# A 128-byte array in front of a fused attention and expert kernel's hid values

## The reference

```python
p = domain_probs / (domain_probs.sum(-1, keepdims=True) + 1e-09)
for e in range(E):
    h = np.maximum(x @ w1[e], 0.0)
    out += p[:, e:e + 1] * (h @ w2[e])
...
h = x @ w_in
g = h * np.cos(h)
return g @ w_out
```

## The kernel before

| array | first byte before | past a multiple of 256 | first byte after | past a multiple of 256 |
|---|---|---|---|---|
| w_hi, w_lo | 16512, 49280 | 128 | same | 128 |
| w_raw, x_hi, x_lo | 82048, 98432, 116864 | 128 | same | 128 |
| hp_hi | 135488 | 64 | 135616 | 192 |
| hp_lo | 141632 | 64 | 141760 | 192 |
| h_raw | 147776 | 64 | 147904 | 192 |
| ident, acc | 153984, 156544 | 128 | 154112, 156672 | 0 |
| t_hi, t_lo | 174976, 184192 | 128 | 175104, 184320 | 0 |
| ex_hi, ex_lo | 193408, 209792 | 128 | 193536, 209920 | 0 |
| attention's q_t, k_t, v_w, prob, prob_t; the cosine's c_u to c_cos | 174976 and on | 128 | 128 more | 0 |

## Time and profile before

### The profile page before, as it was taken

The page is one execution under the profiler, slowest core; times in us unless marked ns, Lnnn a source line. Parts: engine busy times, 40 slices in busy tenths (PEclk is TensorE's granted clock), DMA queues, the critical chain, the costliest instruction groups (busy, mean ns, idle before and its releaser), DMA issues.

```text
span 638.2 us, 10145 instructions
## 1 busy us (share of the span) xinstructions
PE 628.9 (99%) x3656; PEld 562.1 (88%) x3656; DVE 304.4 (48%) x722; ACT 259.6 (41%) x554; POOL 272.9 (43%) x404
## 2 busy tenths in 40 slices
PE   6999999999999999999999999999999999999997
PEld 5887899999899999999998888889999999999996
DVE  6754431215433315433315433426775666766564
ACT  6775322233321223321223321246555467544542
POOL 6883236698720296720296720287000059400000
PEclk9999999999999999999999999999999999999999
DMA  9864100012220021210022210033100002001011
GB/s 281 277 211 153 58 0 1 1 51 82 66 67 1 1 66 66 66 66 0 1 66 67 67 66 1 21 112 100 34 0 1 1 36 98 1 0 49 0 51 50
DMA packets 21896, 37.25 MB, mean 58 GB/s; under 512 B 2784, under 2 KB 14048, under 8 KB 21856
## 3 DMA queue, kind: packets, MB, share of 16 engines
q1 hardware_dynamic: 20688, 36.71, 17.7%
q10 hardware_dynamic: 1168, 0.02, 0.1%
HBM read 34.36 MB, written 2.36 MB: 58 GB/s over the span
## 4 chain that ended last, share of the span: by engine, by line
PE 96%; DVE 2%; ACT 1%; issue 1%; POOL 0%; DVEq 0%
PE bank L1194 31%; PE bank L1166 31%; PE bank L1225 16%; PE bank L1211 14%; PE bank L1158 2%; PE bank L1142 1%; PE bank L1122 1%; DVE s_sb L823 1%; PE bank L1308 1%; ACT prob L574 1%; PE bank L1350 1%; DVE acc L973 0%; DVE prob_t L838 0%; ACT x_hi L587 0%; DVE x_lo L852 0%
## 5 line engine op out<-in xcount | busy, mean ns | idle before, releaser
L424 POOL TENSOR_TENSOR w_lo<-w_raw,w_hi 128x128 fp32r<-128x128 f32 (+1 forms) x252 | 151.2, 636 | 214.7 <-ACT w_hi L606 211.7
L1166 PE MATMUL bank<-x_hi,w_hi 128*128 128x384 f32 (+1 forms) x384 | 131.3, 342 | 0.1
L1166 PE MATMUL bank<-x_hi,w_lo 128*128 128x384 f32 (+1 forms) x384 | 129.0, 336 | 0.0
L1166 PE MATMUL bank<-x_lo,w_hi 128*128 128x384 f32 (+1 forms) x384 | 128.6, 335 | 0.0
L1194 PE MATMUL bank<-w_hi,hp_hi 128*128 128x512 f32 x288 | 114.8, 398 | 0.1
L1194 PE MATMUL bank<-w_hi,hp_lo 128*128 128x512 f32 x288 | 113.4, 394 | 0.0
L1194 PE MATMUL bank<-w_lo,hp_hi 128*128 128x512 f32 x288 | 112.1, 389 | 0.0
L926 DVE TENSOR_TENSOR h_raw<-bank,h_raw 128x384 f32<-128x384 f32 x84 | 46.7, 556 | 91.8 <-PE bank L1211 91.8
L1166 PEld LDWEIGHTS bank<-x_hi,w_hi 128*128 128x128 f32 x384 | 72.1, 188 | 3.3 <-issue 1.0
L1166 PEld LDWEIGHTS bank<-x_lo,w_hi 128*128 128x128 f32 x384 | 72.2, 188 | 1.6
L857 DVE SCALAR_TENSOR_TENSOR hp_lo<-bank,hp_hi 128x384 fp32r<-128x384 f32 x48 | 26.5, 556 | 98.5 <-ACT hp_hi L638 57.5
(11 more groups left out here) (103 smaller groups left out, 965.4 us busy)
## 6 DMA issues: line engine op xcount, KB each, us to landing
w_raw<-in_weights SPq DMA_DIRECT2D x43, 512.0 KB, 3.6
q_t<-in_q SPq DMA_DIRECT2D x12, 192.0 KB, 4.4
result<-acc SPq DMA_DIRECT2D x9, 256.0 KB, 2.1
w_raw<-in_weights SPq DMA_DIRECT2D x8, 256.0 KB, 6.5
k_t<-in_k SPq DMA_DIRECT2D x8, 224.0 KB, 5.3
v_w<-in_v SPq DMA_DIRECT2D x4, 384.0 KB, 5.1
v_w<-in_v SPq DMA_DIRECT2D x4, 320.0 KB, 6.6
k_t<-in_k SPq DMA_DIRECT2D x4, 192.0 KB, 4.0
```

Source lines behind the costliest of these rows:

```text
L424: last = nc.gpsimd.tensor_tensor(w_lo[:, f, at:at + part], raw[:, at - begin:at - begin + part], w_hi[:, f, at:at + part], ALU.subtract)
L1166: last = nc.tensor.matmul(ps[:, 0:TOK], w[:, f, chunk(c)], x[:, c, token_cols(t)], start=c == 0 and i == 0, stop=c == DC - 1 and i == 2)
```

## The change

One array is declared that nothing reads or writes. It takes 128 bytes of every partition, and everything declared behind it moves up by 128 bytes, as the table above shows.

```diff
         p_tok = sb("p_tok", [P, E, TILES])
         half_pi = sb("half_pi", [P, 1])
+
+        sb("apart", [P, 32])
         hp_hi = sb("hp_hi", [P, HP, TOK], F32R)
         hp_lo = sb("hp_lo", [P, HP, TOK], F32R)
         h_raw = sb("h_raw", [P, HP, TOK])
```

## The result

The changed kernel takes 645.46 us (median of 6 runs, 644.92 to 645.97), the kernel before 640.51 us in the same comparison. The ratio is 1.0075, 95% interval 1.0065 to 1.0086. So 128 bytes that nobody reads cost 5.0 us.

What follows compares the result with a forecast made beforehand. TensorE's matmuls were taken to bound the kernel; the terms 0 + 0 + 0 + 0 kept the profiled 640.21 us, and the forecast, 640.4 us, was put between that and the median 640.49; range 637.2 to 643.2 us.

Steps and rivals of the forecast that it cites:

- What bounds the kernel: Whole span: TensorE, busy 99%, binds; the time is a sum over its matmuls, with idle of 0.0 or 0.1 us.
- ACT and DVE: Copies and vector work on these engines: new addresses cost 0; even 10% worse, 55 ns, would be covered by idle time.
- the sums: Up matmuls on `ex` or `t`: 216 get operands 128 apart instead of 0; taken as 0, at most 0.45 us.
- the transfers: Loads at the start and stores at the end: taken as 0, with 0.4 us either way for a tenth.
- the new array: The unused array itself: nothing reads or writes it and no engine gains or loses an instruction, 0 us.
- A shift of 256 is free: Up work: operand starts compared at 384 and 128 past a multiple of 512 gave 173.6 against 173.1 ns.
- Down: 1296 down matmuls, stationary operand from 64 to 192 past a multiple of 256: taken as 0, bounds 2.7 us either way.
- Rival 2: Down and 216 up matmuls: TensorE's two reads collide more; slower, 643.6 us, decided from 1.0 ns per down matmul; chance 0.17.
- 2.1 ns: Down matmuls: time beyond columns that up work lacks, 15.2 against 13.1 ns; the only trace of an address found.
- Loads do cost the stream 13 to 15 ns: TensorE matmuls: argument for more collisions of reads, from 13.1 ns (up) and 15.2 ns (down) beyond the columns.
- The length explains them equally: Down matmuls: streaming 512 columns instead of 384 may explain the extra 2.1 ns as well as the place does.
- The chunk rule: Down weight loads: four chunks 128 bytes apart touch places 64 and 192 before and after, so the move gives 0.

Runs made afterwards that it cites:

- e2: Kernel before with 128 unused bytes behind `h_raw`, so only `acc`, `ex`, `t` and the small arrays move: 640.73 us, ratio 1.0000.
- e3: Kernel before with 128 unused bytes in front of all arrays, so every array moves alike: 640.52 us, ratio 0.9999.
- e9: Kernel before with 256 unused bytes in front of the hid values, everything behind moving too: 640.59 us, ratio 1.0003.
- e1: Kernel before with 128 unused bytes before the hid values and 128 behind `h_raw`, the rest put back: 644.89 us, ratio 1.0071.
- e4: Kernel before with 128 unused bytes before the weights and 128 before the hid values, moving weights and inputs modulo 256: 645.74 us, ratio 1.0084.
- e5: Kernel before with hid values at distance 0 from the weights (modulo 256) instead of 192: 640.45 us, ratio 0.9994.
- e10: Kernel before with hid values 96 behind the weights (modulo 256) instead of 192: 646.79 us, ratio 1.0098.
- e14: Kernel before with only the inputs moved modulo 256, by 64, hid values still 192 from the weights: 642.10 us, ratio 1.0028.
- e6: Kernel before with hid values 32 behind the weights (modulo 256) instead of 192: 645.34 us, ratio 1.0082.
- e17: Kernel before with inputs 64 past the weights and hid values at distance 0 from the weights: 637.21 us, ratio 0.9954.
- e18: Kernel before with inputs 192 past the weights and hid values at distance 0 from the weights (modulo 256): 641.44 us, ratio 1.0017.

## Why the prediction was wrong

- **What bounds the kernel** was read rightly: a sum over TensorE's matmuls, with no wait in it. Of the span's 5.3 us, 5.0 are in the starts of down matmuls.
- **ACT and DVE, the sums, the transfers, the new array**: 0 each, and 0 within what can be told. ACT and DVE moved by 2 ns; up work rose by 0.3 us in the changed kernel and 0.5 in e2, but by 0.4 in e3 too, where no distance changed, so the runs can't tell the 0 for the sums from its bound of 0.45; the stores stayed at 2.0 us. "A shift of 256 is free" was misread, though: in both stretches compared, the two operands begin at the same place modulo 512, so their distance was 0 in both. That was first tested by e9.
- **Down, "I take 0 between these"**, is the step that failed. Its reason was that 64 and 192 lie alike against every multiple of 128, with a grain of 256 left as a possibility. The cost repeats only every 256 bytes (e9 against e1). And the places I compared were the wrong ones: not the stationary operand's against a fixed grid, but its distance from what streams (e3, e4). With that distance changed, the settled pace rose from 228.9 to 233.3 ns, far over the 1.0 ns that was to decide. Rival 2 named that mechanism; I gave it 0.17.
- **Rival 2's price** was too low. I took one more 2.1 ns, from the difference between up and down work. The settled pace rose by 4.4 ns and down work as a whole by 4.96 us / 1296 = 3.8 ns. The 2.1 ns was nearly right as the excess of before over the cheapest pace (2.2 ns), but there was no reason why the next place should cost the same again. The trace of before held the true price: its run from 444.50 us on goes at 233.1 ns (shown above), so the claim of 2.1 ns "in all stretches I looked at" rested on too few stretches. The 0.03 us behind each change from down to up was a weaker hint. "Loads do cost the stream 13 to 15 ns" is shown by no run either: that is what a matmul takes beyond its columns, and every matmul here has a load. The range ended at 643.2 and the result lies 2.3 us above.
- **"The length explains them equally"**: half true. At distance 0 the long stream needs no more than columns and 32 cycles once settled, so the length as such costs nothing. But in e5 a run of 18 pays as much on the way there.
- **The chunk rule.** The Trainium skill ("TensorE: Matmul & The Clock Gate", Weight-path perf modes) has a load read four chunks of 32 columns, here 128 bytes apart, and I had let that speak for no change. If only the places of the chunks counted, a shift of 128 would be free. The runs measure 233.3 against 228.9 ns for it, so the rule is no guide to this cost, whether or not the chunks are read so. With the sentence of the Trainium skill ("TensorE: Matmul & The Clock Gate", Step-by-step) that loading the next weights doesn't steal read bandwidth from the running matmul the runs agree still less: moving what is loaded against what streams, and nothing else, changed the time by up to 1% (e10).

**What stays open.** Shown is that the pace of a run depends on the distance of its two operands' starts modulo 256, on the distances of `hp_hi` and `hp_lo` together, and on what stood ahead of it, and that the plainest paces lie 16 cycles apart, per matmul or per three (544.0, 549.3 and 560.0 cycles). Why is only argued: two reads of the same memory that get in each other's way, and whose relative timing is carried from one matmul to the next, would behave so. No run here sees the memory's inside. Nor does a run show why 0 and 192 are cheap, whether the 32 cycles beyond the columns belong to the load, or why only 45 of the 52 runs of e14 changed their pace. Offsets finer than 32 bytes weren't tried, nor the two halves of the weights apart.

## What to carry to other kernels

When TensorE binds and its stretches are long, measure the distance between starts, in cycles, against columns + 32; an excess that repeats in a fixed pattern may be a layout cost, as it was here, and can be searched for with unused arrays of 32 to 224 bytes at no cost in work. Compare places as the distance between what is loaded and what streams, for each kind of matmul, and measure them together, since a layout that is best for one stretch can spoil how the next is entered. An innocent change of any array's size shifts everything behind it: before a change of under 1% is believed, see whether the starts' pattern in untouched stretches has moved.

## What was not expected of the hardware

- 32 bytes of distance between two operands' starts are worth some 5 us in 640 (e5 against e6: 640.45 and 645.34 us), with no order between neighbours.
- One kernel holds two paces for the same instructions in one execution (e14: 228.9 and 233.3 ns; the kernel before, once behind a pause), and each, once settled, is held to the end of its run.
- A run can need nine matmuls to settle (e5), or three (e17), or none (e18), by what streamed ahead of it.
